# Splitting the first channel product of a retention, MLP and spatial gating chain into seven half-width products by Strassen's scheme

## The reference

```python
# q, k, v: (2 batches, 8 heads, 768 tokens, 64); gamma per head
state = gamma * state + outer(k[t], v[t]);  y[t] = (q[t] @ state) / 8        # retention, 768 steps
x = y as (2, 768, 512)
h = (x^T @ U @ V)^T;  u = x + h                     # U: 768x32, V: 32x768, over tokens
x2 = u + relu(u @ w_ch1) @ w_ch2                    # w_ch1: 512x2048, w_ch2: 2048x512
h = relu(x2 @ w_in)                                 # w_in: 512x1024
a, b = h[:, :512], h[:, 512:]
b = (b - mean(b)) / sqrt(var(b) + 1e-6)
out = (a * (w_spatial @ b + b_spatial)) @ w_out     # w_spatial: 768x768, w_out: 512x512
```

## Time and profile before

| what | value |
|---|---|
| time, 3 runs | 485.6, 485.74, 485.95 us, median 485.74 |
| the profiled execution | 485.74 us, span of the instructions 484.0 us |
| PE busy | 475.5 us (98%), 2744 matmuls, 2744 weight loads |
| DVE, ACT, POOL busy | 202.4, 169.6, 101.9 us |
| granted TensorE clock | 1.000 of full |
| moved by DMA | 33.30 MB; HBM read 29.84 MB |

### The profile page before, as it was taken

How to read it: one execution, slowest core, us unless ns; L and a number is a source line. 1 busy time by engine, 2 the same in 40 slices (tenths; PEclk the granted TensorE clock), 3 DMA queues, 4 the chain that set the end, 5 groups by cost and what they waited for, 6 DMA issues and landing times.

```text
span 484.0 us, 7201 instructions
## 1 busy us (share of the span) xinstructions
PE 475.5 (98%) x2744; PEld 405.7 (84%) x2744; DVE 202.4 (42%) x340; ACT 169.6 (35%) x301; POOL 101.9 (21%) x87
## 2 busy tenths in 40 slices
PE   8899989999999999999999999999999999999997
PEld 5688878888888888888888888888888889999997
DVE  4888886322326543222322541222321775521530
ACT  2534465323336424323333422323331652221212
POOL 2544531232222211232222111232222040000000
PEclk9999999999999999999999999999999999999999
DMA  8999952500000000000000005000002000011003
GB/s 283 373 292 322 323 221 98 250 0 0 0 1 1 0 1 0 0 0 0 0 1 2 0 1 216 12 0 0 0 0 88 0 1 1 1 65 66 0 1 130
DMA packets 8150, 33.30 MB, mean 69 GB/s; under 512 B 832, under 2 KB 2496, under 8 KB 5824
## 3 DMA queue, kind: packets, MB, share of 16 engines
q1 hardware_dynamic: 7712, 32.46, 18.2%
q10 hardware_dynamic: 416, 0.53, 0.3%
HBM read 29.84 MB, written 3.15 MB: 68 GB/s over the span
## 4 chain that ended last, share of the span: by engine, by line
PE 92%; DMA 4%; DVE 1%; SPq 1%; issue 0%; ACT 0%; DVEq 0%
PE bank L1042 10%; PE bank L954 9%; PE bank L955 9%; PE bank L956 9%; PE bank L943 9%; PE bank L944 9%; PE bank L945 9%; PE bank L1057 7%; DMA w2raw<-w 3%; PE bank L968 2%; PE bank L973 2%; PE bank L969 2%; PE bank L1000 2%; PE bank L999 2%; PE bank L998 2%; PE bank L826 2%
## 5 line engine op out<-in xcount | busy, mean ns | idle before, releaser
L340 POOL TENSOR_TENSOR w2l<-w2raw,w2h 128x512 fp32r<-128x512 f32 x48 | 63.7, 1327 | 214.7 <-ACT w2h L445 214.7
L682 DVE SCALAR_TENSOR_TENSOR hl<-bank,hh 128x512 fp32r<-128x512 f32 x48 | 33.2, 691 | 168.1 <-ACT hh L451 168.1
L943 PE MATMUL bank<-uth,w1h 128*128 128x512 f32 x192 | 74.9, 390 | 1.3 <-DVE utl L672 1.3
L945 PE MATMUL bank<-uth,w1l 128*128 128x512 f32 x192 | 74.7, 389 | 0.0
L944 PE MATMUL bank<-utl,w1h 128*128 128x512 f32 x192 | 74.7, 389 | 0.0
L954 PE MATMUL bank<-hh,w2h 128*128 128x512 f32 x192 | 74.7, 389 | 0.0
L955 PE MATMUL bank<-hl,w2h 128*128 128x512 f32 x192 | 74.7, 389 | 0.0
L956 PE MATMUL bank<-hh,w2l 128*128 128x512 f32 x192 | 74.7, 389 | 0.0
L451 ACT ACTIVATE hh<-bank 128x512 fp32r<-128x512 f32 x48 | 28.7, 598 | 89.0 <-PE bank L945 89.0
L445 ACT ACTIVATE w2h<-w2raw 128x512 fp32r (+1 forms) x48 | 30.2, 630 | 67.6 <-PE bank L956 66.3
L943 PEld LDWEIGHTS bank<-uth,w1h 128*128 128x128 f32 x192 | 36.0, 188 | 8.9 <-issue 1.5
(11 more groups left out here) (89 smaller groups left out, 679.8 us busy)
## 6 DMA issues: line engine op xcount, KB each, us to landing
att<-attn SPq DMA_DIRECT2D x7, 1152.0 KB, 7.8
w1raw<-w SPq DMA_DIRECT2D x4, 1024.0 KB, 7.8
w2raw<-w SPq DMA_DIRECT2D x4, 1024.0 KB, 9.2
att<-attn SPq DMA_DIRECT2D x10, 384.0 KB, 5.1
out_T<-stage SPq DMA_DIRECT2D x7, 384.0 KB, 2.3
winraw<-w_in SPq DMA_DIRECT2D x1, 2048.0 KB, 11.4
wsp_raw<-w_sp SPq DMA_DIRECT2D x1, 1920.0 KB, 7.4
tab<-decay SPq DMA_DIRECT2D x7, 258.0 KB, 4.1
```

The source lines that it names most:

```text
L340: nc.gpsimd.tensor_tensor(w2l[k][:, :], w2raw[:, f, :], raw(w2h[k])[:, :], ALU.subtract).then_inc(w2_lo, 1)
L682: nc.vector.scalar_tensor_tensor(out=hl[k][:, :], in0=hid_ps[k][:, :], scalar=0.0, in1=raw(hh[k])[:, :], op0=ALU.max, op1=ALU.subtract).th ...
L943: mm(hid_ps[k][:, :], w1h[k][:, s], uth[t % 2][:, c, :], start=(c == 0), stop=False)
L945: m = mm(hid_ps[k][:, :], w1l[k][:, s], uth[t % 2][:, c, :], start=False, stop=(c == CT - 1))
```

## The change

The hidden tiles are taken in pairs (n = 0 to 23: 3 token tiles x 8 pairs of hidden tiles j and j + 8). The product of a 512 x 256 block of weights and a 512 x 512 block of `u` is seen as one of 2 x 2 blocks (halves of channels, tiles of hidden rows, halves HT = 256 of the tokens) and is formed from seven products of blocks by Strassen's scheme in Winograd's form, instead of eight. Each of the seven is two 128-blocks of channels x 3 matmuls of 256 columns, into parts x, z, y of the two PSUM banks. The operands S of the weights (4 sums a pair, `wsum`) and T of the tokens (4 differences a tile, `tsum`) are formed on DVE or POOL; all seven operands of a pair are rounded and rested (7 instructions each of 256 columns on ACT and DVE, in place of 2 each of 512). The sums of the products that make the four output blocks are partly taken in PSUM, partly by three copies on ACT (`copy_pr`) and three additions on DVE (`sum_c`) a pair.

The weights are no longer kept: `w1` and `w2` are loaded per pair (512 KB each) in all three token tiles. `in_proj(t-1)` stands as one block behind the second pair of tile t. The units of the retention run over all pairs of heads of batch 0 first, then batch 1, and the decay table is loaded for each. The decays of the keys go from POOL to ACT (two activations a unit, but for the first unit), and POOL makes the first pair's sums and rests and the first tile's differences and rests during the retention. The Fori loops are written out. `wsp_raw` is loaded in one piece after the last product.

Core of the diff (`...` where lines are left out):

```diff
+        S_OF = {2: 1, 3: 0, 4: 2, 5: 3}
+        T_OF = {2: 1, 3: 0, 4: 2, 6: 3}
@@ sync
+            for n in range(2, NN):
+                sp.wait_ge(w1_lo, NQ * (n - 1))
+                load_w1(n)
+                sp.wait_ge(w2_lo, 2 * (n - 1))
+                load_w2(n)
+                if n == 3:
+                    sp.wait_ge(u_done, 2 * NI)
+                    sp.dma_start(winraw[:, :, :], w_in).then_inc(win_loaded, 16)
+            sp.wait_ge(pr_done, NQ * NN)
+            sp.dma_start(wsp_raw[:, :, :], w_sp).then_inc(wsp_loaded, 16)
@@ gpsimd
+            for i in range(NI):
+                mask_b(i)
+                if i == 2:
+                    first_weight_sums()
+                elif i == 3:
+                    first_weight_rest(range(0, 4))
+                elif i == 4:
+                    first_weight_rest(range(4, NQ))
+                elif i == 5:
+                    for q in range(4):
+                        token_sum(0, q)
+                elif i == 6:
+                    first_token_rest(range(0, 4))
+            first_token_rest(range(4, NQ))
...
+                    if n:
+                        rest_w2(n - 1, 1)
+                    if t and j == 1:
+                        rstds(t - 1)
+                    rest_w2(n, 0)
+                    if t < NT - 1 and 3 <= j <= 6:
+                        token_sum(t + 1, j - 3)
@@ scalar
+            def decay_k(i):
...
+                for a in range(2):
+                    h = slice(a * DH, (a + 1) * DH)
+                    m = nc.scalar.activation(
+                        kd[k][:, :, h], att[k][:, 2, 0:S - P].rearrange("p (c t) -> p c t", t=P)[:, :, h],
+                        ACT.Copy, scale=tab[k][:, 3 * P + a * DH:3 * P + a * DH + 1])
...
+                xt_copy(i, 0)
+                if i < NI - 1:
+                    decay_k(i + 1)
+                xt_copy(i, 1)
+                if i == 5:
+                    round_b(0, range(0, 2))
+                elif i == 6:
+                    round_b(0, range(2, NQ))
...
+                    copy_pr(n, 0)
+                    if n == 0:
+                        xn_copy(NI - 1, 1)
+                    else:
+                        round_w2(n - 1, 1)
+                    round_w1(n + 1, range(0, 2))
+                    if final:
+                        round_b(t + 1, range(0, 1))
+                    copy_pr(n, 1)
...
+                    round_w1(n + 1, range(2, 4))
...
+                    copy_pr(n, 2)
+                    round_w1(n + 1, range(4, 6))
...
+                    relu_hid(n, 0)
+                    round_w1(n + 1, range(6, 7))
...
+                    relu_hid(n, 1)
+                    round_w2(n, 0)
+                    relu_hid(n, 2)
...
+                    if t == 0 and 3 <= j <= 6:
+                        round_win(j - 3)
@@ vector
+                    if t and j == 1:
+                        add_x2(t - 1, range(CT))
+                    sum_c(n, 0)
+                    if n == 0:
+                        xn_rest(NI - 1, 1)
+                    weight_sums(n + 1, range(0, 3))
+                    rest_w1(n + 1, range(0, 2))
+                    if n == 0:
+                        p_rest(NI - 1)
+                    weight_sums(n + 1, range(3, 4))
+                    if final:
+                        rest_b(t + 1, range(0, 1))
+                    rest_w1(n + 1, range(2, 4))
+                    if final:
+                        rest_b(t + 1, range(1, 2))
+                    sum_c(n, 1)
+                    rest_w1(n + 1, range(4, 5))
+                    if final:
+                        rest_b(t + 1, range(2, 4))
+                    sum_c(n, 2)
+                    if n == 0:
+                        u_add(NI - 1)
+                    rest_w1(n + 1, range(5, 6))
+                    rest_hid(n, 0)
+                    if final:
+                        rest_b(t + 1, range(4, 5))
+                    rest_hid(n, 1)
+                    rest_w1(n + 1, range(6, 7))
+                    if final:
+                        rest_b(t + 1, range(5, 6))
+                    rest_hid(n, 2)
+                    if final:
+                        rest_b(t + 1, range(6, 7))
...
+                    if t == 0 and 3 <= j <= 6:
+                        rest_win(j - 3)
@@ tensor
+            def product(n, q):
+                k = n % 2
+                x, z, y = pr_ps[k][:, 0:HT], pr_ps[1 - k][:, 0:HT], pr_ps[1 - k][:, HT:TW]
+                o = (x, z, x, y, x, y, x)[q]
+                pe.wait_ge(w1_lo, NQ * n + q + 1)
+                if n % NP == 0:
+                    pe.wait_ge(b_lo, NQ * (n // NP) + q + 1)
...
+                if n and q == 0:
+                    pe.wait_ge(c_sum, 3 * n)
+                if n and q == 1:
+                    pe.wait_ge(hid_lo, 3 * n)
+                if q == 2:
+                    pe.wait_ge(pr_copied, 3 * n + 1)
+                if q == 3:
+                    pe.wait_ge(c_sum, 3 * n + 1)
+                if q == 4:
+                    pe.wait_ge(pr_copied, 3 * n + 2)
+                if q == 5:
+                    pe.wait_ge(pr_copied, 3 * n + 3)
+                if q == 6:
+                    pe.wait_ge(c_sum, 3 * n + 2)
+                opens = q in (0, 1, 3)
+                for c in range(2):
+                    s = slice(c * P, (c + 1) * P)
+                    mm(o, w1ch[k][:, q, s], bh[:, q, c, :], start=(opens and c == 0), stop=False,
+                       skip_group_check=True)
+                    mm(o, w1ch[k][:, q, s], bl[:, q, c, :], start=False, stop=False, skip_group_check=True)
+                    m = mm(o, w1cl[k][:, q, s], bh[:, q, c, :], start=False, stop=(c == 1), skip_group_check=True)
+                m.then_inc(pr_done, 1)
...
+                    product(n, 0)
+                    for q in range(1, 7):
+                        product(n, q)
+                        ch2(n - 1, q - 1)
+                    ch2(n - 1, 6)
+                    ch2(n - 1, 7)
+                    if t and j == 1:
+                        in_first(t - 1)
+                        for m in range(2, 2 * CT):
+                            in_group(t - 1, m)
```

More of the change, by code:

```diff
@@ L403, in slot @@
+            for i in range(1, NI):
                 sc_copy(i, 0)
@@ L406, in slot @@
                 sc_copy(i, 1)
[L407 to L409 removed]
+                if i == 2:
+                    round_w1(0, range(0, 2))
+                elif i == 3:
+                    round_w1(0, range(2, NQ))
                 p_round(i - 1)
@@ L525, in round_v @@
+            round_w2(NN - 1, 1)
+            round_x2(NT - 1, range(CT))
             def round_v(m):
@@ L729, in _, with rest_win @@
-            rest_w1(0, 0, 0)
-            xn_rest(NI - 2, 0)
-            xn_rest(NI - 2, 1)
-            mask_a(NI - 1, 1, 1, NI // 2 - 1)
-            states(NI - 1, 0, NC - 2, 1)
-            states(NI - 1, NC - 2, NC - 1, 1)
-            p_rest(NI - 2)
-            rest_u(0, range(0, 3))
-            u_add(NI - 2, NI // 2 - 1, 0)
-            rest_w1(1, 1, 1)
-            rest_u(0, range(3, 4))
+            def rest_win(c):
+                for h in range(2):
+                    s = slice(h * C, (h + 1) * C)
+                    dve.wait_ge(win_hi, 2 * c + h + 1)
+                    nc.vector.tensor_tensor(winl[:, c, s], winraw[:, c, s], raw(winh)[:, c, s],
+                                            ALU.subtract).then_inc(win_lo, 1)
@@ L961, in in_proj @@
-            def in_proj(t):
-                xh, xl = uth[t % 2], utl[t % 2]
+            kv(0, 0, NC - 2)
+            scores(0, 1)
+            kv(0, NC - 2, NC - 1)
+            outputs(0, 0)
+            outputs(0, 1)
+            for i in range(1, NI):
+                scores(i, 0)
+                turn(i - 1, 0)
+                turn(i - 1, 1)
+                scores(i, 1)
+                kv(i, 0, NC - 2)
+                kv(i, NC - 2, NC - 1)
+                down(i - 1)
+                outputs(i, 0)
+                outputs(i, 1)
+                up(i - 1)
@@ L1029, in _ @@
-            in_proj(NT - 1)
+                        mm(o, winh[:, c, w], x2h[:, c, :], start=(c == 0), stop=False)
+                        mm(o, winh[:, c, w], x2l[:, c, :], start=False, stop=False)
+                        last = mm(o, winl[:, c, w], x2h[:, c, :], start=False, stop=(c == CT - 1))
+                last.then_inc(in_done, 1)
+            turn(NI - 1, 0)
+            product(0, 0)
+            product(0, 1)
+            turn(NI - 1, 1)
+            product(0, 2)
+            product(0, 3)
@@ new lines, in _ @@
+            down(NI - 1)
+            product(0, 4)
+            product(0, 5)
+            up(NI - 1)
+            product(0, 6)
+            for t in range(NT):
+                for j in range(NP):
+                    n = t * NP + j
+                    if n == 0:
+                        continue
+                    product(n, 0)
[4 more added lines that the diff above has]
+                    ch2(n - 1, 7)
```

(9 more changed lines are left out.)

877 lines of the change are left out of this document (438 added, 439 removed).

## The result

The changed kernel takes **486.96 us** (median of 20 runs) against 485.63 for the kernel before (20 runs): ratio 1.0023, 95% interval 1.0014 to 1.0033. It is slower by a small amount that is larger than the uncertainty. The profiled execution took 486.92 us, span 485.1: 1.18 us and 1.1 us more than the one of before. The time lies in the range that was given, but the sum came out on the other side: +1.2 in place of -0.6.

A forecast was written before the change was run, and what follows sets the result against it. PE's matmul rate was taken as the bound (PE busy 98%). Terms -9.4 -0.4 +4.9 +2.9 +0.7 +0.2 +0.5 = -0.6 gave 485.1 us from 485.74, called no change; range 478.5 to 493.

The forecast's parts named there:

- the one on pair 0: Pair 0 and start of pair 1: PE waits 0.75, 0.3 and 3.15, less an earlier wait of 1.3: +2.9 us.
- The walk: Instruction-by-instruction timing of one pair on DVE, ACT and POOL: last hidden rest at 10.95, wanted at 11.19.
- rival 1: DVE mostly goes first and POOL waits: last pairs lose 0.7 each, pair 0 1.6 net; 479 us, chance 0.26.
- the last pairs: Last pairs of tiles 0 and 1: seven extra `rest_b` on DVE make PE wait 2.45 each, +4.9 us.
- the small terms: `rest_win` in tile 0 +0.7, second pairs of tiles 1 and 2 +0.2, late `wsp_raw` loads +0.5 us.
- the retention: Before the channel products: slot 2's mask earlier -2.1, slots 5 and 6 +0.3, slot 7 +1.4; together -0.4 us.
- the product: Seven-product scheme over 24 pairs: 256-column matmuls at 0.120 save 0.39 a pair, second product kept at 5.43: -9.4 us.
- rival 2: Products' 256-column matmuls spaced 0.114 to 0.116 in place of 0.120; 481 us, chance 0.10.
- Plain pairs keep up: In a plain pair of 10.47 us the other engines finish in time: 0 cost, 0.24 us to spare.
- rival 3: DVE with POOL bounds every pair, P1 waiting 0.4 in some 20 pairs: +8, 493 us, chance 0.19.
- Rival 4: Streamed weights come late if 1 MB takes over 10.7 us; 514 us at 12 us, chance 0.05.
- `rest_win` and `wsp_raw`: Pairs 3 to 6 of tile 0 +0.7; `wsp_raw` loads landing after the last product +0.5 us.

The follow-up runs named there:

- e1: Changed kernel with pair 0's w2 rounded on ACT in slot 7 of the retention and rested on POOL ahead of the channel products: 484.0 us, ratio 0.9968.
- e6: Changed kernel with POOL's w2 rests cut to 8 of 512 columns, so the result lacks that low part: 480.06 us, ratio 0.989.
- e2: Changed kernel with 14 unused 512-column matmuls filling PE's wait between the first two products of pair 1: 484.84 us, ratio 0.9987.
- e7: Kernel before the change with only the key decays of units 1 to 7 moved from POOL to ACT: 484.77 us, ratio 0.9978.
- e4: Changed kernel with three of ACT's five `round_b` moved from slot 6 to slot 7 of the retention, behind the scores' copy: 485.55 us, ratio 0.9998.
- e9: e5 plus ACT rounding the previous pair's second w2 half before its first copy, so POOL's rest can start sooner: 483.19 us, ratio 0.9944.
- e3: Changed kernel with two more of DVE's `rest_b` put behind the last hidden rest in the last pair of a tile: 487.79 us, ratio 1.0056.
- e5: Changed kernel with the edits of e1 and e4, and DVE's last `u_add` behind pair 0's last hidden rest: 481.24 us, ratio 0.9913.
- e8: e5 plus five unused 512-column matmuls between the first two products of pair 1: 481.85 us, ratio 0.9922.

## Why the prediction was wrong, point by point

**The step that failed** is the one on pair 0: "P1 [waits] 3.15 for the last hidden rest ... **+2.9**". The place, the releaser and the kind of wait were right; the size was not. The wait is 4.16, because POOL's two rests of `w2` fall back to back onto a hidden rest and a weight rest there and cost 2.1 (e1, e6). The walk had room for one: rival 1, in which POOL holds nothing, prices pair 0 at 1.6 in place of 2.9, one rest less. DVE's own queue was sized about right: 3.15 less 1.3 is 1.85, and 2.03 is left in e1 and e6. The two waits in pair 0 are 0.79 (forecast 0.75) and 0.69 (0.3). Above all, the sum ends at the wait: it has no term for the clock. PE with 0.37 us of work in 4.3 comes back at half the clock, and that costs 2.3 more (e2: 2.1 by itself). With +4.2 and +2.3 in place of +2.9 the forecast would have been +3.0, over the measured +1.2. That the time still fell inside the range is in good part luck: the last pairs (-1.4), the small terms (-1.3), the retention (-0.2) and the product (+1.0) were wrong by -1.9 together.

**The product: -8.4 in place of -9.4.** The matmuls of 256 columns are spaced 0.119, a little better than the 0.120 chosen between the bounds. The loss is in the ones of 512 columns behind them:

```profile
114.87 0.28 PE L1123 MATMUL bank<-bh,w1cl 128*128 128x256 f32 x1
114.99 0.40 PE L1136 MATMUL bank<-hh,w2h 128*128 128x512 f32 x1
115.22 0.40 PE L1138 MATMUL bank<-hl,w2h 128*128 128x512 f32 x1
115.46 0.39 PE L1139 MATMUL bank<-hh,w2l 128*128 128x512 f32 x1
115.68 0.28 PE L1120 MATMUL bank<-bh,w1ch 128*128 128x256 f32 x1
```

The starts in the records are 0.234, 0.236 and 0.228 apart in a block behind seven-product matmuls, against 0.227 of the earlier trace rows: 0.018 a block, six blocks a pair, 23 pairs make 2.5 us, of which the first matmul of 256 behind each block, spaced 0.116, gives 0.4 back. The prediction kept the second product at its 5.43. The Trainium skill (TensorE: Matmul & The Clock Gate, section Back-to-back issue gap) gives 109 ns for 256 columns; the measured 119 is 10 above, as the 227 is above its 216, so rival 2, which leaned that way, is out.

**Plain pairs keep up: right.** The walk put the last hidden rest 10.95 into the pair; in the pair that starts at 113.55 it begins at 124.14 and ends at 124.55, 11.0 into it. The slack of about 0.2 held, and rival 3 (a wait in every pair) did not come. Rival 4 did not either: 5.0 us to landing against 10.7 allowed. Rival 1 (DVE mostly first) is wrong in the plain pairs and in pair 0 and right at 156.23.

**Last pairs: +3.5 in place of +4.9.** The wait is named DVE `hl` as forecast, and is 1.44 and 1.39 over a matmul's spacing in place of 2.45. The walk had laid both of POOL's rests on DVE; at 156.23 DVE was first and POOL stood. The Trainium skill (SBUF — State Buffer, section Who interferes with whom) calls it an exclusive lock, which a DVE instruction with at most one SBUF input does not need; the trace agrees, with 1.54 for 0.41 on DVE where POOL was first, 2.63 for 1.30 on POOL where DVE was, and 0.41 for a DVE instruction with an input in PSUM. The rule tells who stands only with starts known to 0.1 us, and a walk doesn't have them. In tile 0 a further 0.36 is in the last pair itself: P5 is 0.20 late behind ACT's `copy_pr 2`, which stands behind two `round_b` of 0.62, and only 0.08 comes before P6, for which `sum_c 1` was forecast "just in time".

**Retention: -0.56 in place of -0.4**, each term close: slot 2's mask 1.9 earlier (forecast 2.1, 1.3 of it by the decays on ACT, e7), nothing lost in slots 5 and 6 (0.3), 1.36 given back in slot 7 (1.4, e4). **`rest_win` and `wsp_raw`**: nothing in place of 1.2. DVE took the two rests of `win` with POOL's difference beside (2.05 for 1.3 at 113.94) and still met its next sum, which shows slack there of at least 0.7; e9 shows where it ends.

**What stays open:** why the 512-column matmuls are slower behind those of 256, and what gave the other 0.6 us of the retention.

## What to carry to other kernels

A wait on the engine that bounds the kernel is priced as the wait and the clock behind it: here 4.2 us of wait cost 2.1 to 2.3 more, and what a shorter one costs differs from run to run. When an engine with slack gets a second one's neighbour to share with (DVE and POOL both on SBUF operands), count the pairs of instructions that can meet and look first at the places with no slack; there, moving POOL's instructions out (e1) pays, and moving DVE's own work (e3) or POOL's a little (e9) only changes who meets whom. The algorithm's saving of 8.4 us was real and was spent at two seams, the first pair and the change of tile; mending the first seam and the last slot of the retention (e5) turned 0.23% slower into 0.87% faster.

## What the hardware showed that was not expected

- PE granted 0.51 of its clock for 5.1 us behind a wait of 4.2; behind a gap of 2.15 (start to start, like those that follow) with 0.8 and 0.9 ahead of it (e1) 0.58 for 2.7 us and 0.71 for 2 more; behind three of 1.05, 1.24 and 1.33 (e5) the full clock.
- The same waits do not cost the same in every run. The changed kernel's 20 runs have 0.993 (one 0.992) of the clock over the span in ten (median 487.4 us) and 0.996 in the other ten (486.3). With the gap of 2.15, six of ten runs are at 0.996 in e1 and one of six in e6; e8 shows half clock in one of six with nothing before it but 1.03 and 1.24.
- POOL pays for the shared way too: a rest takes 1.30 us, or 1.46 to 2.63 where DVE stood in an instruction with SBUF inputs as it started.
- Matmuls of 512 columns directly behind those of 256 are 0.234 and 0.236 apart, and back at 0.228 by the third; the first of 256 behind them follows at 0.116.
